# Attention and two MLPs on one core: the fully-masked flag taken from the row sum on GpSimd, and P·V of a pair of heads in four groups instead of nine

## The reference

```python
def _attn_ref(q, k, v, tau):                      # (4, 8, 576, 64)
    scale = 1.0 / np.sqrt(q.shape[-1])
    scores = scale * np.matmul(q, k.transpose(0, 1, 3, 2))
    thresh = np.max(scores, axis=-1, keepdims=True) - tau      # tau = 0.02
    scores = np.where(scores >= thresh, scores, -1000000000.0)
    scores = scores - np.max(scores, axis=-1, keepdims=True)
    attn = np.exp(scores)
    attn = attn / (np.sum(attn, axis=-1, keepdims=True) + 1e-09)
    return np.matmul(attn, v)
# then x = attn_out as (2304, 512)
# layer 1: h = x @ w_in;  r = max(h, 0);  (s*r*r + b) @ w_out            d_ff = 2048
# layer 2: h = x @ w_in2; (max(h, 0) + alpha*min(h, 0)) @ w_out2         d_ff = 2048
```

## Time and profile before

| | value |
|---|---|
| median of 3 runs | 1148.56 us |
| the profiled execution | 1148.55 us, span 1146.8 us |
| PE busy | 1115.7 us (97%) |
| DVE busy | 560.1 us (49%) |
| ACT busy | 516.8 us (45%) |
| POOL busy | 260.3 us (23%) |
| mean granted TensorE clock | 0.997 |
| attention stage | from 0 to about 337 us of the span |

### The profile page before, as it was taken

One profiled execution on the slowest core, in us unless ns is written; L12 is line 12 of the kernel. 1 busy time (PEld: TensorE's weight loads), 2 busy tenths in 40 slices (PEclk: granted clock), 3 DMA queues, 4 the chain that ended last, 5 costly groups with the idle time before them and its releaser, 6 DMA issues.

```text
span 1146.8 us, 19091 instructions
## 1 busy us (share of the span) xinstructions
PE 1115.7 (97%) x5881; PEld 884.2 (77%) x5881; DVE 560.1 (49%) x1088; ACT 516.8 (45%) x925; POOL 260.3 (23%) x440
## 2 busy tenths in 40 slices
PE   5899999999999999999999999899999999999998
PEld 4666766666668888888888889888888888888887
DVE  6799999989953333233233225632332232232232
ACT  4577777777764432232232225633333333243243
POOL 3455555555545420000000005900000000000000
PEclk9899999999999999999999999999999999999999
DMA  6555656555501110000000003500000000000010
GB/s 155 134 141 128 147 125 144 129 139 134 131 11 55 46 37 0 0 0 0 0 0 0 0 0 94 164 1 1 0 37 0 0 37 0 0 37 0 0 38 19
DMA packets 100118, 59.75 MB, mean 52 GB/s; under 512 B 67040, under 2 KB 83440, under 8 KB 100080
## 3 DMA queue, kind: packets, MB, share of 16 engines
q1 hardware_dynamic: 100080, 59.28, 20.4%
HBM read 30.94 MB, written 4.72 MB: 31 GB/s over the span
## 4 chain that ended last, share of the span: by engine, by line
PE 89%; SPq 5%; issue 2%; ACT 1%; DVE 1%; DMA 1%; DVEq 0%; ACTq 0%
PE psum L833 23%; PE psum L834 23%; PE psum L835 23%; PE psum L939 6%; PE psum L855 4%; PE psum L912 4%; SPq L367 3%; PE psum L857 2%; SPq L343 1%; PE psum L841 1%; PE psum L909 1%; PE psum L920 1%; SPq L346 1%; DMA k_low_half<-k_lo 0%; DMA q_both<-q_lo 0%
## 5 line engine op out<-in xcount | busy, mean ns | idle before, releaser
L833 PE MATMUL psum<-x_hi,win_hi 128*128 128x512 f32 (+1 forms) x640 | 239.2, 374 | 1.9 <-DVE x_lo L764 1.9
L834 PE MATMUL psum<-x_lo,win_hi 128*128 128x512 f32 (+1 forms) x640 | 238.8, 373 | 0.0
L835 PE MATMUL psum<-x_hi,win_lo 128*128 128x512 f32 (+1 forms) x640 | 238.7, 373 | 0.0
L833 PEld LDWEIGHTS psum<-x_hi,win_hi 128*128 128x128 f32 x640 | 120.7, 189 | 25.6 <-DVE x_lo L764 3.1
L835 PEld LDWEIGHTS psum<-x_hi,win_lo 128*128 128x128 f32 x640 | 120.6, 188 | 23.0
L834 PEld LDWEIGHTS psum<-x_lo,win_hi 128*128 128x128 f32 x640 | 120.8, 189 | 22.8
L782 DVE SCALAR_TENSOR_TENSOR act_r<-act_n,nalpha,act_r 128x512 f32<-128x512 f32 (+1 forms) x80 | 55.9, 698 | 159.3 <-ACT act_r L625 159.0
L774 DVE SCALAR_TENSOR_TENSOR g_lo<-act_r,b_c,g_hi 128x512 fp32r<-128x512 f32 (+1 forms) x80 | 60.6, 758 | 134.1 <-ACT g_hi L617 134.1
L696 DVE TENSOR_REDUCE negm<-psum 128x1 f32<-128x576 f32 x144 | 108.5, 754 | 34.2 <-PE psum L857 27.3
L771 DVE SCALAR_TENSOR_TENSOR act_r<-act_r,s_c 128x512 f32<-128x512 f32 (+1 forms) x80 | 67.8, 848 | 116.2 <-ACT act_r L614 116.2
L491 POOL TENSOR_SCALAR ex<-ex,none_in,rinv 128x576 f32<-128x576 f32 x144 | 118.2, 821 | 24.0 <-DVE rinv L724 22.5
(11 more groups left out here) (81 smaller groups left out, 1591.1 us busy)
## 6 DMA issues: line engine op xcount, KB each, us to landing
k_twice<-k_hi SPq DMA_DIRECT2D x64, 144.0 KB, 2.5
stage<-in_moe_w_out_dram SPq DMA_DIRECT2D x32, 256.0 KB, 2.7
k_low_half<-k_lo SPq DMA_DIRECT2D x32, 144.0 KB, 2.5
out_dram<-stage SPq DMA_DIRECT2D x18, 256.0 KB, 2.2
raw_q<-in_q_dram SPq DMA_DIRECT2D x32, 128.0 KB, 2.4
raw_k<-in_k_dram SPq DMA_DIRECT2D x32, 128.0 KB, 2.5
raw_v<-in_v_dram SPq DMA_DIRECT2D x32, 128.0 KB, 2.7
q_both<-q_hi SPq DMA_DIRECT2D x32, 128.0 KB, 2.3
```

Of the source, the lines that this page charges most:

```text
L833: nc.tensor.matmul(dst, lhs[0], rhs[0], start=first, stop=False)
L834: nc.tensor.matmul(dst, lhs[0], rhs[1], start=False, stop=False)
L835: return nc.tensor.matmul(dst, lhs[1], rhs[0], start=False, stop=final)
```

## The change

Two edits are made.

1. `nothing_left` is gone from DVE, and `extra` is gone. `all_masked` on POOL now computes `none_in` from the row sum: 1e-9/576 where the row sum is at most 0, else 0. It runs one step later than before and waits for the mask of the tile. The denominator is the row sum plus 1e-9, by one `tensor_scalar` on DVE, and waits for no other engine. `normalise` waits for POOL's own flag.
2. `PV` has four entries (steps 11, 13, 18 and 20, with 2, 3, 2 and 3 pieces) in the place of nine, and the first output copy goes one step earlier.

```diff
+        GUARD = 1e-9
-        PV = {10: [(0, 0)], 11: [(0, 1)], 13: [(0, 2)], 14: [(0, 3)], 15: [(0, 4)],
-              18: [(1, 0), (1, 1)], 19: [(1, 2)], 20: [(1, 3)], 21: [(1, 4)]}
+        PV = {11: [(0, 0), (0, 1)], 13: [(0, 2), (0, 3), (0, 4)],
+              18: [(1, 0), (1, 1)], 20: [(1, 2), (1, 3), (1, 4)]}
-        FIRST_OUT, SECOND_OUT = 15, 21
+        FIRST_OUT, SECOND_OUT = 14, 21
@@ all_masked (POOL)
-                wait_alone(pool, none_ok, t.twos + 1)
-                nc.gpsimd.tensor_scalar(extra[r, t.cols], none_in[r, t.cols], float(S), 1e-9, ALU.mult,
-                                        ALU.add).then_inc(extra_ok, 1)
+                wait_alone(pool, normed, t.count - TPP + 1)
+                wait_alone(pool, freed, t.uses + 1)
+                nc.gpsimd.tensor_scalar(none_in[r, c], rsum[r, c], 0.0, GUARD / S, ALU.is_le, ALU.mult).then_inc(none_ok, 1)
@@ normalise (POOL)
+                wait_alone(pool, none_ok, t.twos + 1)
@@ emit (POOL)
-                if t.tile and t.closes:
-                    all_masked(t)
+                if before.tile and before.closes:
+                    all_masked(before)
@@ denominator (DVE); nothing_left and its call are removed
-                wait_alone(dve, extra_ok, t.twos + 1)
-                nc.vector.tensor_tensor(den[r, c], rsum[r, c], extra[r, c], ALU.add).then_inc(den_ok, 1)
+                nc.vector.tensor_scalar(den[r, c], rsum[r, c], GUARD, None, ALU.add).then_inc(den_ok, 1)
```

More of the change, by code:

```diff
@@ L111, in attention_mlp_mlp @@
         none_in = sb("none_in", [P, TPP], where=att)
-        extra = sb("extra", [P, TPP], where=att)
         rsum = sb("rsum", [P, TPP], where=att)
@@ L161, in attention_mlp_mlp @@
         none_ok = sem("none_ok")
-        extra_ok = sem("extra_ok")
         den_ok = sem("den_ok")
@@ L481, in all_masked @@
             def all_masked(t):
-                r = slice(0, P)
-                wait_alone(pool, none_ok, t.twos + 1)
-                nc.gpsimd.tensor_scalar(extra[r, t.cols], none_in[r, t.cols], float(S), 1e-9, ALU.mult,
-                                        ALU.add).then_inc(extra_ok, 1)
+                r, c = slice(0, P), t.cols
+                wait_alone(pool, normed, t.count - TPP + 1)
+                wait_alone(pool, freed, t.uses + 1)
+                nc.gpsimd.tensor_scalar(none_in[r, c], rsum[r, c], 0.0, GUARD / S, ALU.is_le, ALU.mult).then_inc(none_ok, 1)
             def normalise(t):
                 r, c = slice(0, P), t.col
+                wait_alone(pool, none_ok, t.twos + 1)
                 wait_alone(pool, rinv_ok, t.twos + 1)
@@ L494, in emit @@
             def emit(n0, l):
-                t, after, normed_now = Use(n0, l), Use(n0, l + 1), Use(n0, l - NORM_LAG)
+                before, after, normed_now = Use(n0, l - 1), Use(n0, l + 1), Use(n0, l - NORM_LAG)
                 if normed_now.tile:
@@ L750, in emit @@
                     mask(t)
-                if after.tile and after.closes:
-                    nothing_left(after)
                 if before.tile and before.closes:
```

## The result

The changed kernel takes 1152.31 us (median of 10 runs, 1150.56 to 1153.0) against 1148.84 us before (10 runs, beside it on the same chip). The ratio is 1.0027, 95% interval 1.0018 to 1.0036: slower by 3.5 us. The forecast was 1152.8. Of the runs further down, one of flag_only (1230.09 us) and one of cover (2797.95 us) lie far off all others and are left out of their figures.

A forecast was written before the change was run, and what follows sets the result against it. It took a pair as bound by the key DMA chain, then PE's work. Stalls over savings, 0.25 us a pair (3.5 us), plus 0.8 drain and nothing for the flag gave +4.3: 1152.8 us, 8-in-10 range 1143 to 1157.

The forecast's parts named there:

- The wait at the fill of tile 0: PE's one wait per pair, put on the DMA of `k_low_half`, not on DVE's mask as the profile mostly names.
- part A: Pair's stretch from the end of tile 5's scores to the next pair's fill of tile 0: 8.49 us, unchanged.
- The wait itself: PE's wait at the fill of tile 0, to grow from about 0.4 to about 0.9 us.
- What the groups save: Fewer entries and exits of P·V on PE: 1.00 us saved per pair in Part B.
- Part B: Rest of a pair, from the fill of tile 0 on, PE never waiting before: 10.96 us, to become 11.21.
- What the stalls cost: Three PE waits for ACT's copies of the single `turned` bank in Part B: 0.35, 0.33 and 0.57, together 1.25 us.
- The third: Stall from turn of step 15 to tails of step 16, set by ACT's order: 0.57 us, 0.32 from `FIRST_OUT` = 14.
- The drain: Stretch after the last fill of tile 0: +0.8 us, between -0.5 and +1.5.
- The flag at nothing: Removing `nothing_left`, 2.7 us of DVE per pair, was to change the time by nothing.
- the gain comes through: Rival: DVE bounds the wait at the fill, so the kernel gets faster, 1127.5 us, or 1145 with stalls; chance 0.06.
- the held `den`: Rival: POOL holds DVE's `den` ahead of the K chain, 0.3 us per pair, 4 us more, 1156.8 us; chance 0.10.
- Saved switches and stalls cancel: Rival: the two cancel within 0.15 us a pair, giving 1147 to 1150.5 us; chance 0.20.

The follow-up runs named there:

- flag_only: The kernel before with only the flag edit, P·V still in nine groups: 1149.13 us, ratio 1.0009.
- cover: The changed kernel with P·V in seven groups (steps 10, 11, 14, 15, 18, 19, 21) and the first output copy at step 15: 1146.77 us, ratio 0.9987.
- cover_oldflag: cover with `k_hi` moved ahead of ACT's turn copy and exponential, and the flag made on DVE as before: 1141.80 us, ratio 0.9936.
- pv_only: The kernel before with only P·V in four groups and the output copy at step 14, old flag kept: 1150.59 us, ratio 1.0020.
- first15: The changed kernel with only the first output copy back at step 15: 1150.08 us, ratio 1.0016 to the kernel before.

## Why the prediction was right, and where it was not

**The wait at the fill of tile 0 is the DMA's, and part A is fixed.** Right, and shown from both sides. Part A is 8.49 us before and after, although PE has two groups less in it, and it moves when ACT's order is moved.

**The wait itself** was to grow from 0.4 us to 0.9. It grew from 0.46 to 0.60. Two terms were mis-sized. PE's work in part A falls by 0.5 (0.31 of P·V, 3 × 0.69 to 1.76, and 0.20 of one exit) and not by 0.7: the group ahead of the fill had no price on leaving that could be saved, since the fill behind it waits in any case and takes 0.39 before and after. And 0.37 come back as a stall at the turn of step 8, with one score tile between it and the turn before. The rows are those of the changed kernel, ACT and PE:

```profile
207.22 0.59 ACT L566 COPY pt<-psum 128x512 f32<-128x512 f32 x1 [0.81 <-PE psum L901]
...
207.87 0.66 PE L901 MATMUL psum<-ident,ex 128*128 128x128 f32 x4
```

This cost no time here, since the landing covers it.

**What the groups save.** The entries and exits came as read: P·V of 8 and 12 matmuls took 1.01 and 1.45 us. Part B had 1.00 us less of PE's work.

**What the stalls cost.** All three are there. Turn 11 ends 214.88 - 213.55 = 1.33 after the tails turn (1.32 forecast), for 0.97. From turn 14 to turn 15 it is the same cycle: turn 15 starts at 220.84 in the timeline and ends at 221.50, 1.33 behind 220.17. The chain doesn't go over it; from turn 14 on it follows ACT to the tails. The third was too large: from the end of turn 14 (220.17) to the end of the tails (222.89) it takes 2.72, and I had 2.86. The exponential there starts at 0.78 (0.82 forecast), and the copy follows 0.63 behind its start, not 0.75: ACT starts the next copy before the exponential's full duration is over. That is the term that was mis-sized: 0.43 for the forecast 0.57, or about 0.1 us a pair. A pair costs +0.15, where I had +0.25.

**`FIRST_OUT`.** I put 0.32 us of the third stall on it. Taken away alone it gives 0.06. The price of the instruction was right, but I had looked at one wait, and ACT's next waits took the rest.

**The drain.** +0.8 forecast. From the last fill of tile 0 (306.82 and 310.22) to the first matmul of layer 1 (337.49 and 341.32) it was 30.67 before and 31.10 after: +0.4.

**The flag at nothing.** Right for the steady pair: flag_only has the same one. Over the whole kernel its median is 1 us above before, at the edge of what can be told from nothing. It is right only because the DMA chain and PE's work cover it, as cover_oldflag shows.

**The sum.** Undisturbed, the changed kernel is 2.5 us slower (1151.08 against 1148.55, both profiled): 2.0 in the pairs, 0.4 in the drain. The median is 3.5 us higher. A late landing in most executions would make up the difference, which is not shown. So the forecast of 4.3 us came near the median partly by luck: terms that were too large (3.5 for 2.0 in the pairs, 0.8 for 0.4 in the drain) met something that it did not have. The direction and the mechanism were right.

**The rival "the gain comes through"** fell with pv_only and flag_only, the held `den` with its mean of 158 ns: the 128x2 form can be held, as its one meeting with POOL shows, but it does not meet POOL in the steady pairs. "Saved switches and stalls cancel" was nearest among the rivals: first15 is close to it.

## What to carry to other kernels

Work that separates two users of a single buffer isn't only cost: before it is gathered elsewhere, count what each gap needs (here 1.32 us from turn to turn, of which 0.66 are the copy and its hand-over). Where a wait's name and the code disagree, look for an occurrence at which the named engine was late: one such row gave the DMA chain, and one copy moved in another engine's order then gave more (7 us) than all the regrouping.

Take engine work away when the engine is the limit: the same flag edit is worth nothing in the kernel before and 4 us in the fastest version here.

## What the runs showed of the hardware that was not expected

- A set of score matmuls (128x288) directly behind another set begins with 0.33 us in the chain, like one behind P·V, and with 0.13 us behind transposes.
- The copy behind an exponential on ACT starts 0.63 us after the exponential's start, although the exponential is recorded with 0.75 us.
- A DMA of 144 KB from SBUF to SBUF that lands in 2.5 us landed in 3.9 us in one profiled execution, with the same instructions, and not in another.
- A `den` of one source on DVE took 0.14 us as 128x1 while POOL's normalisation ran, once in every pair. As 128x2, which takes 0.16 us alone, it took 0.34 us and ended with POOL's instruction. The old `none_in`, with two sources in SBUF, ended with POOL's instruction too, and so did the old two-source `den` even as 128x1 (0.26 us, 212.89 to 213.15, where POOL's ends at 213.14).
